# One pass for the top-32 mask: a parametric rectifier in place of a rectifier and a subtraction, and transposes and value products one slot earlier

## The reference

```python
scores = scale * np.matmul(q, k.transpose(0, 1, 3, 2))
kth = np.partition(scores, -top_k, axis=-1)[..., -top_k:-top_k + 1]
scores = np.where(scores >= kth, scores, -1000000000.0)
scores = scores - np.max(scores, axis=-1, keepdims=True)
attn = np.exp(scores)
attn = attn / (np.sum(attn, axis=-1, keepdims=True) + 1e-09)
attn_out = np.matmul(attn, v)
...
gate = 1.0 / (1.0 + np.exp(-gate_pre))          # gate_pre: 5-tap causal convolution of x
x = gate * (x @ w_val) @ w_out
...
u = x + np.real(fft(fft(x, axis=1), axis=2))
un = (u - mu) / np.sqrt(var + 1e-06)
out = u + np.maximum(un @ w_ch1, 0.0) @ w_ch2    # 512 -> 2048 -> 512
```

## Time and profile before

| | |
|---|---|
| time, median of 3 runs | 1214.94 us (1213.46 to 1216.52) |
| time of the profiled execution | 1222.09 us |
| its span, first to last instruction | 1220.3 us |
| PE busy | 1053.3 us (86%) |
| DVE busy | 917.6 us (75%) |
| ACT busy | 606.4 us (50%) |
| POOL busy | 555.9 us (46%) |
| mean granted clock of PE | 0.926 |

### The profile page before, as it was taken

How to read it: one execution, slowest core, us unless ns; L and a number is a source line. 1 busy time by engine, 2 the same in 40 slices (tenths; PEclk the granted TensorE clock), 3 DMA queues, 4 the chain that set the end, 5 groups by cost and what they waited for, 6 DMA issues and landing times.

```text
span 1220.3 us, 20060 instructions
## 1 busy us (share of the span) xinstructions
PE 1053.3 (86%) x6608; PEld 836.8 (69%) x6608; DVE 917.6 (75%) x2044; ACT 606.4 (50%) x1253; POOL 555.9 (46%) x704
## 2 busy tenths in 40 slices
PE   2776557589989999989798999989798999998998
PEld 2555445465578888866487888866587888647887
DVE  6999999997999897797988989797997980320000
ACT  3777656544556555544456655544565554012221
POOL 2666655343545445353645545444554443133221
PEclk9896765798989899999899999999899999998999
DMA  9476366020257666520356756321366656306974
GB/s 250 154 210 204 110 198 204 11 67 8 78 182 245 201 228 214 186 76 1 118 197 211 261 206 216 128 74 45 101 225 209 232 180 207 108 1 229 351 279 161
DMA packets 81190, 200.39 MB, mean 164 GB/s; under 512 B 8384, under 2 KB 26560, under 8 KB 81088
## 3 DMA queue, kind: packets, MB, share of 16 engines
q1 hardware_dynamic: 81088, 199.11, 48.8%
HBM read 177.58 MB, written 21.50 MB: 163 GB/s over the span
## 4 chain that ended last, share of the span: by engine, by line
PE 61%; DVE 20%; issue 9%; POOL 5%; ACT 3%; DMA 1%; SPq 1%; DVEq 0%; ACTq 0%; POOLq 0%
PE p_m L555 17%; PE p_m L569 17%; PE p_m L463 13%; DVE rest L747 8%; DVE top L753 6%; PE p_t L436 5%; PE p_t L452 4%; PE p_s L423 4%; DMA u<-w_ch 1%; DVE gate L793 1%; POOL k_lo L882 1%; ACT prob L638 1%; POOL prob L893 1%; DVE gv L840 1%; POOL q_st L880 1%
## 5 line engine op out<-in xcount | busy, mean ns | idle before, releaser
L893 POOL TENSOR_TENSOR prob<-s_sb,prob 128x576 f32<-128x576 f32 x144 | 206.4, 1433 | 237.4 <-ACT prob L631 237.4
L753 DVE MAX8 top<-rest 128x8 f32<-128x576 f32 x432 | 304.7, 747 | 0.0
L747 DVE MATCH_REPLACE8 rest<-top,rest 128x576 f32<-128x576 f32 x288 | 211.7, 743 | 0.0
L569 PE MATMUL p_m<-w_st,hid_hi 128*128 128x512 f32 x640 | 203.9, 400 | 0.2 <-POOL hid_lo L957 0.2
L555 PE MATMUL p_m<-un_hi,w_st 128*128 128x320 f32 (+1 forms) x1024 | 172.5, 312 | 35.5 <-POOL un_lo L948 21.4
L555 PEld LDWEIGHTS p_m<-un_hi,w_st 128*128 128x128 f32 x1024 | 149.0, 197 | 46.3 <-POOL un_lo L948 22.3
L436 PE MATMUL p_t<-id_sb,prob 128*128 128x128 f32 x720 | 121.3, 304 | 64.0 <-ACT or_sb L655 37.1
L957 POOL TENSOR_TENSOR hid_lo<-hid,hid_hi 128x256 fp32r<-128x256 f32 (+1 forms) x128 | 106.6, 833 | 148.7 <-ACT hid_hi L695 148.7
L631 ACT ACTIVATE prob<-s_sb,bias 128x576 f32<-128x576 f32 x144 | 111.0, 771 | 109.6 <-POOL bias L889 109.5
L625 ACT ACTIVATE s_sb<-p_s 128x576 f32<-128x576 f32 x144 | 93.0, 646 | 131.7 <-PE p_s L423 131.6
L423 PE MATMUL p_s<-k_hi,q_st 128*128 128x512 f32 (+1 forms) x320 | 116.3, 366 | 35.4 <-POOL k_lo L882 16.6
(11 more groups left out here) (80 smaller groups left out, 1604.4 us busy)
## 6 DMA issues: line engine op xcount, KB each, us to landing
w_st<-w_split SPq DMA_DIRECT2D x256, 512.0 KB, 4.5
w_split<-w_st SPq DMA_DIRECT2D x32, 512.0 KB, 3.0
q_raw<-qT SPq DMA_DIRECT2D x64, 144.0 KB, 3.7
k_raw<-kT SPq DMA_DIRECT2D x64, 144.0 KB, 3.7
u<-w_ch SPq DMA_DIRECT2D x32, 256.0 KB, 3.7
v_sb<-v SPq DMA_DIRECT2D x16, 256.0 KB, 3.7
wslot<-w_val SPq DMA_DIRECT2D x4, 1024.0 KB, 5.8
wslot<-w_out SPq DMA_DIRECT2D x4, 1024.0 KB, 5.3
```

The source lines that it names most:

```text
L569: mm = pe.matmul(mbank(j), h[i % 2][:, P * j:P * j + P], w2_st[i % NB2][:, w, :], start=f == 0 and part == 0, stop=f == FC - 1 and part == 2)
L747: dve.match_replace(rest[tt % 2][:, :], top[tt % 4][:, 8 * n - 8:8 * n], src[:, :], LOWEST).then_inc(s_chain, 1)
L753: found = dve.max(top[tt % 4][:, 8 * n:8 * n + 8], rest[tt % 2][:, :])
L893: pool.tensor_tensor(prob[t % 3][:, 0:S], s_sb[t % NS][:, :], prob[t % 3][:, 0:S], ALU.subtract).then_inc(s_arg, 1)
```

## The change

A mask pass less: ACT now computes a parametric rectifier with slope 2^-100 on its negative side. Of the value 2^100 * (kth - s) it keeps the huge positive one for a dropped score, and gives -(s - kth) for a kept one; the exponential follows with the scale negated and scale * (kth - max) as its bias. The subtraction on POOL (L893) is gone. POOL makes the two biases with two instructions in place of one, and the factors tile with its two memsets is gone. Rectifier and exponential of a tile now stand in the same slot (s-4), the exponential behind a wait for the rectifier on the same engine. The reciprocal and the transposes come at lag 5 (they were at 6) and the value product at lag 6 (it was at 7); as the mixing steps start at a slot that `ATTEND` sets, each of them comes one slot earlier as well. The convolution taps and the tanh keep their slots, and so do splits, loads and selection.

```diff
-FILLS = 19
+FILLS = 17
-SELECT, PENALTY, EXPONENT, RECIP, TRANSPOSE, ATTEND = 1, 4, 5, 6, 6, 7
+SELECT, EXPONENT, RECIP, TRANSPOSE, ATTEND = 1, 4, 5, 5, 6
...
                 def copy_scores(t):
                     act.wait_ge(s_qk, t + 1)
                     if t >= NS:
-                        act.wait_ge(s_arg, t - NS + 1)
+                        act.wait_ge(s_drop, t - NS + 1)
...
-                def penalty(t):
-                    act.wait_ge(s_bias, t + 1)
+                def exponent(t):
+
+                    act.wait_ge(s_bias, 2 * (t + 1))
                     if t >= 3:
                         act.wait_ge(s_tr, t - 2)
-                    act.activation(prob[t % 3][:, 0:S], s_sb[t % NS][:, :], ACT.Relu,
-                                   bias=bias[t % 4][:, 1:2], scale=-BIG).then_inc(s_pen, 1)
-
-                def exponent(t):
-                    act.wait_ge(s_arg, t + 1)
+                    act.activation(prob[t % 3][:, 0:S], s_sb[t % NS][:, :], ACT.Prelu,
+                                   bias=bias[t % 4][:, 1:2], scale=-BIG, alpha=1.0 / BIG).then_inc(s_drop, 1)
                     if t >= 4:
                         act.wait_ge(s_radd, t - 3)
+                    act.wait_ge(s_drop, t + 1)
                     act.activation(prob[t % 3][:, 0:S], prob[t % 3][:, 0:S], ACT.Exp,
-                                   bias=bias[t % 4][:, 0:1], scale=SCALE,
+                                   bias=bias[t % 4][:, 0:1], scale=-SCALE,
                                    accum_out=psum_row[:, t % 4:t % 4 + 1]).then_inc(s_exp, 1)
...
-                    if due(s, PENALTY):
-                        penalty(s - PENALTY)
                     if due(s, EXPONENT):
                         exponent(s - EXPONENT)
...
-                                dve.wait_ge(s_bias, tt - 3)
+                                dve.wait_ge(s_bias, 2 * (tt - 3))
...
-                dve.memset(factors[:, 0:1], -SCALE).then_inc(s_zero, 1)
-                dve.memset(factors[:, 1:2], BIG).then_inc(s_zero, 1)
...
-                    pool.tensor_tensor(bias[t % 4][:, :], top[t % 4][:, 0:TOPK:TOPK - 1], factors[:, :], ALU.mult).then_inc(s_bias, 1)
-
-                def argument(t):
-                    pool.wait_ge(s_pen, t + 1)
-                    pool.tensor_tensor(prob[t % 3][:, 0:S], s_sb[t % NS][:, :], prob[t % 3][:, 0:S], ALU.subtract).then_inc(s_arg, 1)
+                    most, kth = top[t % 4][:, 0:1], top[t % 4][:, TOPK - 1:TOPK]
+                    pool.tensor_scalar(bias[t % 4][:, 1:2], kth, BIG, None, ALU.mult).then_inc(s_bias, 1)
+                    pool.tensor_scalar(bias[t % 4][:, 0:1], kth, most, SCALE, ALU.subtract, ALU.mult).then_inc(s_bias, 1)
...
-                    if due(s, PENALTY):
-                        biases(s - PENALTY)
-                        argument(s - PENALTY)
+                    if due(s, EXPONENT):
+                        biases(s - EXPONENT)
```

More of the change, by code:

```diff
@@ L132, in build @@
         id_sb = sb("id_sb", [P, P])
-        factors = sb("factors", [P, 2])
         power = sb("power", [P, 1])
@@ L199, in build @@
         s_bias = sem("s_bias")
-        s_pen = sem("s_pen")
-        s_arg = sem("s_arg")
+        s_drop = sem("s_drop")
         s_exp = sem("s_exp")
```

## The result

| | before | after |
|---|---|---|
| median of 15 runs, same chip | 1215.45 us (1213.38 to 1221.77) | 1222.11 us (1217.28 to 1225.38) |
| profiled execution | 1222.09 us, span 1220.3 | 1223.37 us, span 1221.6 |
| ratio of the times | 1 | 1.0039 (95% interval 1.0022 to 1.0056) |

The kernel became slower by 0.39%, 4.7 us of 1215. The time lies in the range that was given, 6.8 us above the forecast, and not within the 0.3% that was forecast. The two medians lie 6.7 us apart because the runs of after fall in two groups, seven up to 1219.1 and eight from 1222.1 on, and the median is the lowest of the upper one; the ratio is the better figure. The runs of before have the same two groups, but only two of the 15 are in the upper one (1221.5 and 1221.8 us).

The account below looks back on a forecast made before the run. DVE's selection was taken to bound the kernel up to 242 us, PE from 276.3 us. Terms -2.7 - 2.2 - 2.5 + 4.8 + 1.2 + 1.8 = +0.4 us gave 1222.5, less 7.15 for the median: 1215.3 us, range 1205 to 1223.

Parts of the forecast that it names:

- the sum: All gains and losses of the change added up: +0.4 us on the profiled execution's 1222.09 us.
- The relief: Gains from dropping POOL's subtraction and mixing a slot earlier: 2.7, 2.2 and 2.5 us.
- The taps: DVE's twelve convolution taps before 242 us get faster without POOL's subtraction: 2.7 us gained, bounds 0 and 5.4.
- The move of the mixing: `zed` 2 of batch 0 goes ahead of a selection part at the DVE-bound part's end: 2.2 us gained, once.
- the 0.6 us for each of batches 1 and 2: Faster taps right ahead of `zed` 2, 1.3 us, less 0.7 us: 0.6 us gained in each of these batches.
- The collision: Split now shares a slot with `trn` 1 and first hidden chunk: stall 8.6 us for 7.0, 4.8 us lost over three.
- The added work: Second bias 0.25 us and exponential's wait 0.15 us a tile, exposed in split slots: 1.2 and 1.8 us lost.
- The slower clock: Half-speed PE clock behind a stall, 5.1 us of work lost; only Rival (b) counted it.
- Rival (b): Eight stalls behind splits grow 3.2 us beyond the sum, plus 5.1 us of slower clock: 1223.6 us, chance 0.24.
- The offset: The profiled execution took 7.15 us more than the median; taken off 1222.5, it gave 1215.3 us.
- (a): Relief counts and collision doesn't, all 5.4 us on DVE come back: 10.1 us faster, 1204.8 us, chance 0.27.
- (c): Parametric rectifier needs another activation table than the exponential, two loads a tile on ACT: near 1340 us, chance 0.03.

Follow-up runs that it names:

- `mask_only`: The changed kernel with the lags of before (reciprocal and transposes at 6, value product at 7), so the mixing starts where it did before; 0.9995 of before.
- experiment 1: The group of runs with `before_small_sub` and `mask_only`; the cited lengths of a batch stretch are 265.90 us in before and 266.18 in `before_small_sub`.
- `bias_first`: The changed kernel with POOL making the biases of a slot ahead of its share of the split instead of behind it; 0.984 of before.
- `trn_first`: `bias_first`, and in a split slot that begins with a `trn` step ACT and POOL do that step first; 0.979 of before.
- `mask_one_bias`: `mask_only` with the single bias instruction of before in place of two; 0.9951 of before.
- `one_bias`: The changed kernel with the single bias instruction of before in place of two; 1.0053 of before.
- second execution of before: The kernel before, unchanged, profiled a second time; 1217.3 us, span 1215.5.
- `before_bias_first`: The kernel before with POOL's biases ahead of its share of the split, the subtraction staying behind it; 0.9888 of before.
- `before_small_sub`: The kernel before with POOL's instruction on 2 of 576 columns, as an addition, and the exponential's scale negated; 0.9933 of before.

## Where the prediction held and where it failed, step by step

The time, 1222.11 us, lies in the range of 1205 to 1223, near its upper end. That isn't the merit of the sum, which had +0.4 us: like with like (upper group against upper, lower against lower) the change costs some 3 us, and the sum was right in its parts and their signs but short in the losses.

**The relief: right in all, its terms not.** `zed` 2 of batch 0 was forecast at 268.7 us and starts at 269.71. The taps gave 12 x (1.272 - 0.883) = 4.7 us before 242 us, where I had taken half of the excess, 2.7, with 5.4 as the bound. The move of the mixing was forecast at 2.2 us: `zed` 2 starts at 270.05 us in `mask_only`, 0.34 later than in after, with twelve taps that took 815 ns and so 0.8 us less in all, which leaves about 1.1, an estimate. And the 0.6 us for each of batches 1 and 2 didn't come (265.90 and 266.18 us in experiment 1). The rule of the Trainium skill (SBUF — State Buffer, "SBUF: two separate sides"), an exclusive lock for a VectorE operation with two SBUF inputs, has its direction in these rows: the two-input tap speeds up and the one-input MAX8 stays at 747 ns. Its size, a whole subtraction for each tap, isn't there.

**The collision: right mechanism, too small.** A stall of 8.6 us was forecast, 9.13 came, three times. From the transposes to the bias 5.57 us passed (5.5 forecast), from the bias to the chunk 4.77 (4.5 forecast). So the loss is 2.1 x 3 = 6.3 us and not 4.8. `mask_only` has 7.58 us in this place without the collision, so 0.5 us of the 2.1 are the added work and 1.5 the collision. `bias_first` and `trn_first` show that what PE waits for there is the order of bias, split and normalised rows on ACT and POOL.

**The added work: too small, and in more places.** I took 0.25 us for the second bias, by the mean of the one it replaces, and 0.15 for the exponential's wait. The chain shows 0.44 and 0.18, 0.62 us together. The stall of the earlier trace rows grew by 1.3 us where 0.9 was forecast, that of the earlier trace rows by 0.6 for 0.4 in batch 0 and by less later. Besides, PE now waits 0.30 and 0.42 us for the exponential in two more slots of a batch (312 and 416 us), in which I had called the added work hidden; in before it doesn't. Under the lags of before the second bias alone is worth 5.3 us by the ratios (`mask_one_bias`), for 1.2 us of the sum and a part of the 1.8. This is the step of the sum that failed: the instruction is short, but it stands in the chain that ends each split slot's stall, and its price there is its issue and its length, not the mean of another one. In after itself the 5.3 us can't be had back by taking the instruction out (`one_bias`), so for the changed kernel only the stalls give its price.

**The slower clock: left out of the sum.** With the losses of the collision and the added work, less the taps' gain in batches 1 and 2, the sum had 6.6 us of idle time behind `zed` 2; 9.15 came. It had 1.5 us of busy time, the owed scores; 4.4 came. So 2.5 us are mis-sized stalls and 2.9 us are matmuls that ran slower, in an execution of the upper group. Rival (b) had this term with 5.1 us, for a stall of about 10 us. That was misread: in the 10.24 us of the earlier trace rows PE was busy for 5.17, and half the clock costs it half of these, 2.6 us. The stall of 9.13 us overlaps in after with a stretch at 0.50, 1.2 GHz, with 5.55 us of busy time in it, and the sum should have held what it adds:

```profile
328.57:338.81 10.24, 5.55 (x24) 5.36 (x25) 7.22 (x16) 4.25 (x9) 2.96 (x6) 0.50 0.15 49
```

In before the stretch there lasted 6.8 us, with 3.34 us of busy time (first execution, from 337.06 us). Rival (b) came nearest by its time, 1223.6, and by its mechanism, a dearer second bias and more time at the lower clock; the sizes are in part luck, as with 2.6 for 5.1 it has 1221.1.

**The offset.** The sum stood on the profiled execution and I took off 7.15 us as if that were a constant. 5.5 us of it were the first stretch's matmuls at the lower clock, in an execution that most runs of before don't resemble (two of the 15 lie that high). Of after's runs eight of 15 lie in their upper group. So 1222.5 for the profiled execution met 1223.37 by luck: that execution of before held 5.5 us of slower matmuls which the sum didn't know of, and against the second execution of before the change costs 6.1 us of span and not 0.4.

**Rivals (a) and (c).** The relief of (a) is real, 0.9933 by itself, but the other two parts took it back. (c) fell. Groups of instructions over the whole span of after:

```profile
L613 ACT ACT_TABLE_LOAD x1 | 1.3, 1283 | 2.2 <-DVE power L853 2.2
```

One load, as in before, so the parametric rectifier lies in the set of the exponential. The list of that set in the Trainium skill (ScalarE: Activation LUTs, "Table sets: the hidden batching unit") has tanh and relu in it; the trace adds this one.

## What to carry to other kernels

When work goes from an engine that doesn't bound, ask what stands in its queue ahead of the small operation for which others wait: here the place of a small bias instruction behind a split of 2.8 us cost 13.6 us (`before_bias_first`), the 144 subtractions 8.1 (`before_small_sub`). Another order for the steps of a slot was worth more than the pass that was taken away. Price an added instruction by the chain that ends the stall, from its releaser's end to the start of what waits for it. Before a sum is made against one profiled execution, compare it with the median: an execution above it may hold work at a lower clock that isn't an offset.

## What was unexpected in the hardware

- PE of the same kernel, with the same idle time to 0.02 us in each stretch, took 5.5 us more for its matmuls behind `zed` 2 in one execution than in another (spans 4.8 us apart), by stretches at half clock in different places; for `trn_first` it is 12 us between two groups of runs. What decides which of them come wasn't found.
- POOL's two-input subtraction of 128x512 takes 1.27 us alone, 1.69 and 2.56 us beside DVE's two-input operations, and DVE's `k_lo` beside POOL's takes 1.94 us for 0.74. Getting one engine to the same point earlier can so cost what it gains.
- POOL's instructions on one column (278 and 329 ns on the mean, 0.61 us beside DVE's share of the split) are no cheaper than one on two columns (245).
- An activation that waits for the one ahead of it on its own engine starts 0.86 us behind the start of that, and 0.68 without the wait.
